# Two weight-chunk loads, their upper parts and eight matmuls moved at the first expert tile of an attention, MoE and MLP kernel

## The reference, cut to what matters

```python
# 1: attention, B=4, H=8, S=768, D=64: a window of 128 keys and 4 sink keys
a = softmax(where(is_sink | in_window, q @ k.T / sqrt(D), -1e9)); x = a @ v      # x: 3072 rows of 512
# 2: skip or route each row to the best of 8 experts (D=512, F=1024)
do_compute = x @ w_skip > 0
e_idx = argmax(x @ w_gate); gate_w = softmax(x @ w_gate)[e_idx]
out = x + gate_w * (relu(x @ w1[e_idx]) @ w2[e_idx])       # rows with do_compute; the others stay x
# 3: an MLP of 2048 on all 3072 rows
y = relu(out @ w_in) ** 2 @ w_out
```

## Time and profile before

| | |
|---|---|
| median of three runs | 923.6 us (923.23 to 924.84) |
| time of the profiled execution, and its span | 924.56 us, 923.1 us |
| PE busy, PE weight load busy | 898.7 us (97%), 730.4 us (79%) |
| DVE, ACT, POOL busy | 471.5 us (51%), 421.6 us (46%), 81.4 us (9%) |
| chain that ended last, share of PE | 90% |
| granted TensorE clock, mean over the span | 0.996 of full |

### The profile page before, as it was taken

How to read it: one execution, slowest core, us unless ns; L and a number is a source line. 1 busy time by engine, 2 the same in 40 slices (tenths; PEclk the granted TensorE clock), 3 DMA queues, 4 the chain that set the end, 5 groups by cost and what they waited for, 6 DMA issues and landing times.

```text
span 923.1 us, 16966 instructions
## 1 busy us (share of the span) xinstructions
PE 898.7 (97%) x5152; PEld 730.4 (79%) x5153; DVE 471.5 (51%) x1418; ACT 421.6 (46%) x971; POOL 81.4 (9%) x147
## 2 busy tenths in 40 slices
PE   7999999979999998999999999999999999999998
PEld 5778777758788886878888888888888888888886
DVE  5787899875776667764242224222422342243224
ACT  7888899854666666553132113221312231232123
POOL 3112221223111111100000000000000000000000
PEclk9999999999999999999999999999999999999999
DMA  5556775285666768640003002100400040004001
GB/s 200 168 161 200 231 240 169 75 292 204 221 247 250 245 242 308 246 109 0 1 36 57 1 1 65 26 0 0 91 0 0 0 91 0 0 0 91 0 0 45
DMA packets 87364, 99.52 MB, mean 108 GB/s; under 512 B 56093, under 2 KB 56221, under 8 KB 87312
## 3 DMA queue, kind: packets, MB, share of 16 engines
q1 hardware_dynamic: 81168, 83.34, 28.8%
q0 software_dynamic: 6000, 15.49, 4.9%
q10 hardware_dynamic: 144, 0.07, 0.0%
HBM read 77.72 MB, written 25.56 MB: 112 GB/s over the span
## 4 chain that ended last, share of the span: by engine, by line
PE 90%; DMA 2%; issue 2%; ACT 2%; DVE 2%; ACTq 1%; DVEq 0%; SPq 0%; POOLq 0%
PE bank L1154 28%; PE bank L1140 28%; PE bank L1033 7%; PE bank L1052 7%; PE bank L892 5%; PE bank L947 4%; PE bank L920 4%; PE bank L958 1%; PE bank L1041 1%; DMA w_raw<-in_weights 1%; PE bank L972 1%; ACT w_hi L788 1%; PE bank L940 1%; PE bank L1025 1%; ACTq L786 1%
## 5 line engine op out<-in xcount | busy, mean ns | idle before, releaser
L1523 DVE TENSOR_TENSOR g<-relu_c 128x512 f32<-128x512 f32 x96 | 66.4, 692 | 340.7 <-ACT relu_c L835 340.7
L835 ACT ACTIVATE relu_c<-bank 128x512 f32<-128x512 f32 x96 | 57.4, 598 | 371.7 <-PE bank L1140 371.7
L1140 PE MATMUL bank<-x_hi,w_lo 128*128 128x512 f32 x384 | 149.6, 390 | 0.7 <-DVE x_lo L1510 0.7
L1154 PE MATMUL bank<-w_hi,g_lo 128*128 128x512 f32 x384 | 150.3, 391 | 0.0
L1154 PE MATMUL bank<-w_lo,g_hi 128*128 128x512 f32 x384 | 149.6, 390 | 0.0
L1154 PE MATMUL bank<-w_hi,g_hi 128*128 128x512 f32 x384 | 149.5, 389 | 0.0
L1140 PE MATMUL bank<-x_lo,w_hi 128*128 128x512 f32 x384 | 149.5, 389 | 0.0
L1140 PE MATMUL bank<-x_hi,w_hi 128*128 128x512 f32 x384 | 149.5, 389 | 0.0
L679 ACT ACTIVATE prob<-score,neg_max 128x264 f32<-128x264 f32 (+1 forms) x192 | 94.0, 495 | 14.7 <-DVE neg_max L1216 14.6
L1482 DVE TENSOR_TENSOR w_lo<-w_raw,w_hi x70 | 82.0, 1221 | 23.9 <-ACT w_hi L788 23.8
L1154 PEld LDWEIGHTS bank<-w_hi,g_lo 128*128 128x128 f32 x384 | 72.1, 188 | 17.4 <-DVE g_lo L1530 2.5
(11 more groups left out here) (150 smaller groups left out, 1278.4 us busy)
## 6 DMA issues: line engine op xcount, KB each, us to landing
w_raw<-in_weights SPq DMA_DIRECT2D x80, 512.0 KB, 5.5
k_in<-in_kT SPq DMA_DIRECT2D x24, 264.0 KB, 3.7
q_in<-in_qT SPq DMA_DIRECT2D x24, 256.0 KB, 3.2
v_in<-in_v SPq DMA_DIRECT2D x24, 256.0 KB, 3.9
x_rows<-x_row SPq DMA_DIRECT2D x24, 256.0 KB, 3.1
x_row<-x_rows SPq DMA_DIRECT2D x96, 64.0 KB, 2.5
out<-w_raw SPq DMA_DIRECT2D x12, 512.0 KB, 2.9
x_res<-routed POOLq DMA_DIRECT2D x15, 260.0 KB, 3.3
```

What stands on the lines that cost most here:

```text
L1140: ins = eng.matmul(hc_ps[f % 2][:, :], w[f // UNIT][:, f % UNIT, wcols], x[:, c, :], start=(c == 0 and n == 0), stop=(c == DC - 1 and n == 2))
L1154: ins = eng.matmul(yc_ps[s][:, :], gg[:, f % 2, s * P:(s + 1) * P], w[f // UNIT][:, f % UNIT, DM:CH], start=(f == 0 and n == 0), stop=(f = ...
L1523: eng.tensor_tensor(g[:, f % 2, :], relu_c[:, f % 2, :], relu_c[:, f % 2, :], ALU.mult).then_inc(s_cg, 1)
```

## The change

Three places are changed. SP loads chunks 6 and 7 of unit 1 behind the load of tile 1's rows, instead of behind the store of the last row tile. ACT makes the upper parts of chunks 3 to 5, then `x_upper(1)`, then chunks 6 and 7, instead of 3 to 6, `x_upper(1)`, 7. PE does the eight third terms of tile 0's layer 2 before it turns tile 1's rows, instead of after.

```diff
@@ block.sync
-                if i == TILES + 1:
-                    for f in range(6, UNIT):
-                        eng.wait_ge(s_wlo, f + 1)
-                        load_chunk(1, f)
...
             eng.wait_ge(s_pad0, 16)
             eng.wait_ge(s_bturn, 2)
             eng.dma_start(x_raw[:, :], routed[P:2 * P, :]).then_inc(s_bx, 16)
+            for f in range(6, UNIT):
+                eng.wait_ge(s_wlo, f + 1)
+                load_chunk(1, f)
@@ block.scalar, first_tile
-                for f in range(3, 7):
+                for f in range(3, 6):
                     upper_chunk(1, 1, f, s_whi)
                 x_upper(1)
-                upper_chunk(1, 1, 7, s_whi)
+                for f in range(6, UNIT):
+                    upper_chunk(1, 1, f, s_whi)
@@ block.tensor, tile
                 layer2((4, 5, 6, 7), (0, 1))
+                layer2(range(FC), (2,))
                 if drain:
                     turn_x(n + 1)
-                layer2(range(FC), (2,))
```

## The result

The change makes the kernel slower: 927.94 us median of 11 runs (925.79 to 931.19) against 924.01 us (923.20 to 924.88), ratio 1.0044 with a 95% interval of 1.0031 to 1.0056. Forecast were 925.7 us and +2.1; measured are +3.9, and +4.3 against the 923.6 us from which the prediction started, so about twice the forecast. Run once more beside the kernel before, 12 times, it took 927.08 against 924.29, ratio 1.0027 (1.0015 to 1.0039), +2.8. So the direction and the place were right, and the size was forecast too small. The profiled execution took 928.32 us, its span 926.9.

What follows compares the result with a forecast made beforehand. PE, busy 97% of the span, was taken as the bound, so its waits and low-clock stretches move the end. A 0.4 us later layer 1 plus 1.7 for the clock gave +2.1 on 923.6: 925.7 us, range 923.0 to 928.0.

Steps and rivals of the forecast that it cites:

- Third terms ahead of the turn: On PE, tile 0's eight third terms would run from 202.80 to 204.6 at full clock, in formerly idle time.
- The scatter: Stage 1's last scatter would land in 3.0 us instead of 5.56, without 1 MB of weights in flight.
- The rival that it doesn't get faster: The last scatter's 5.56 us are its own or the padding stores'; 928.2 us in total, chance 0.15.
- ACT held by `s_wtail`: Before chunk 4 ACT waits for all four tail chunks, so tile 1's rows wait for 1 MB of weights.
- The rival that ACT isn't held: Chunks 6 and 7 land before ACT needs chunk 4; layer 1 starts near 207, 919.9 us, chance 0.05.
- The landing, T + 6.1: Chunks 6 and 7 land 6.1 us after tile 1's rows are asked for, bounds 5.3 and 6.5.
- free for the same reason as the chunks: SP's next loads, for unit 2, stand behind chunks 6 and 7 and were taken to cost nothing.
- T: Time at which SP asks for tile 1's rows: 201.5 forecast, bounds 201.1 and 202.6, instead of 204.02.
- The clock, 1.7: After PE's wait before layer 1 of tile 1, a stretch at 1.2 GHz would lose 1.7 us.
- The rival in which the clock holds: Clock stays up until layer 1 of tile 1, so only 0.4 us stays: 924.0 us, chance 0.18.
- Each us by which layer 1 of tile 1 starts late or early is a us of the total: From 210.71 to the end of tile 1 PE has no wait, so start shifts pass fully into the total.
- The sum: Layer 1 of tile 1 starts 0.4 us late, at 211.1, plus 1.7 for the clock: +2.1 us.

Runs made afterwards that it cites:

- e3_own_sem: Changed kernel, but chunks 6 and 7 of unit 1 count up their own semaphore, awaited only behind tile 1's upper part; 922.44 us, ratio 0.9982 to the kernel before.
- e10_x_first: Changed kernel with the upper part of tile 1's rows made right behind chunk 3, ahead of ACT's wait for the tail; 923.87 us, ratio 0.9996 to the kernel before.
- e13_changed_again: The changed kernel unaltered, run once more beside the kernel before; 927.08 us against 924.29, ratio 1.0027.
- e1: Kernel before with only SP's loads of chunks 6 and 7 moved behind tile 1's rows; 929.52 us, ratio 1.0048.
- e5: Changed kernel, with SP holding unit 2's first loads until unit 1's four tail chunks have landed; 927.32 us, ratio 1.0044 to the kernel before.
- e12: Changed kernel with chunk 5 too moved behind tile 1's rows, three loads instead of two; 928.44 us, ratio 1.0056 to the kernel before.
- e14: Changed kernel with SP holding unit 2's first loads until the tail has landed, run a second time; 926.79 us, ratio 1.0024 to the kernel before.
- e9_act_only: Kernel before with only ACT's order changed, chunk 6's upper part behind that of tile 1's rows; 923.95 us, ratio 1.0003.
- e16_hold_and_fill: Changed kernel with unit 2's first loads held and 20 idle matmuls behind the turn; 924.45 us, ratio 1.0005 to the kernel before.
- e4_fill: Changed kernel with 20 idle matmuls on PE behind the turn of tile 1's rows; 928.02 us, ratio 1.0037 to the kernel before.
- e6_fill_longer: Changed kernel with 29 idle matmuls on PE behind the turn of tile 1's rows; 926.93 us, ratio 1.0036 to the kernel before.

## Why the prediction was right in direction and short in size

- **Third terms ahead of the turn: right.** They run with no wait behind terms 0 and 1. Moved alone they give 1.7 us in the median, with an interval that reaches 1.0000.
- **The scatter: right.** 3.0 us forecast, 2.86 measured. Over the profiles it takes 2.74 to 3.16 in nine with the chunks behind it, and 4.83 to 5.56 in four where they still lead. The rival that it doesn't get faster is out.
- **ACT held by `s_wtail`: right, and shown.** Taking only this wait away gives 5.5 us back (e3_own_sem); moving one instruction ahead of it gives 4.1 (e10_x_first). The rival that ACT isn't held is out.
- **The landing, T + 6.1: the step that failed.** This term of the sum was mis-sized. It measured 7.7 in the profiled run, outside the bounds of 5.3 and 6.5, and 7.1 in the mean of eight profiles. The prediction called SP's next loads "free for the same reason as the chunks". They run beside the tail (the DMA engines are busy to 0.94 from 203.0 to 210.5) and delay it: with them held it measures 6.0 to 6.4, the value forecast. With T half a microsecond later than forecast (202.02, from the scatter's later start) and ACT 0.1 quicker, it makes layer 1 start at 213.00 and not 211.1.
- **The clock, 1.7: mis-sized too.** One dip was forecast, as after the wait before; in all six profiles in which PE idles some 5 to 8 us in front of layer 1 (after, e13_changed_again, e1, e5, e12 and e14) the clock stays low for twice as long. In the profiled run 2.3 us were lost, in e13_changed_again 2.1. This lay inside the bound of 2.5. The rival in which the clock holds is out.
- **"Each us by which layer 1 of tile 1 starts late or early is a us of the total": wrong for what is won.** With the hold 2.0 us become 0.6, by the low clock and the next weights; with the own semaphore 4.3 become 1.7, by the next rows and the next weights.
- **The next weights: chance, as far as known.** Expert 1's first tile waits 0.91 us in place of 0.26. The sum had no term for it, but e9_act_only, with loads and PE as before, waits 0.93 there.
- **The sum.** 0.4 + 1.7 = 2.1 was forecast (its upper bounds, 1.9 and 2.5, lead to 928.0 and not to the 927.6 that it names). The profile has 2.3 for the start of layer 1, 2.3 for the clock and 0.6 for the weights, 5.2 at 245 us, less a good 1 for the dip that isn't there near 355. That landing and clock together make the loss is shown by e16_hold_and_fill: without both it is 0.2 over before (interval 0.9988 to 1.0021). The 2.6 us can't be divided by adding up the two corrections, 0.3 and 0.7: without the other, the low clock takes half of what the hold wins, and the idle matmuls themselves hold layer 1 up. What makes +3.9 in one set of runs and +2.8 in another of the same kernel stays open.

## What to carry to other kernels

A semaphore that counts a group of loads makes the first member wait for the last: before a load of the group is moved later, look for the wait that counts it and for everything queued behind that wait on its engine. Whoever moves such a load parts the semaphore, which here turned a loss of 0.3 to 0.4% into a gain of 0.18%. And a wait that is taken off PE is worth only as much as the next limit leaves; here the next tile's rows and the next expert's weights took back 2.6 of 4.3 us.

## What was not expected of the hardware

The clock fell to 1.2 GHz although PE had run 4.83 us of dense matmuls, idled only 2.03 us and was 1.4 us into dense matmuls again (e4_fill). With 1.10 us of idling behind as long a filler (e16_hold_and_fill), and with none (e6_fill_longer), it didn't. So filling most of a wait bought nothing in the median, and filling nearly all of it kept the clock.

Loads that are issued later on the same engine's queue can delay earlier ones. The two chunks reached ACT 6.0 to 6.4 us after the issue of the rows just ahead of them when SP held its next three loads of 512 KB, and 6.1 to 8.2 us (7.1 in the mean of eight profiles) when it didn't.
